# Batch 0's attention in two half batches of plain float32 products, and weights laid out tile by tile

## What is computed

```python
# attention, 8 heads of 64; a query sees itself and the 127 tokens before it
scores = q @ k.T / 8 - slope[h] * |i - j|         # masked outside the window
attn = softmax(scores);  x = concat_heads(attn @ v)            # (4, 576, 512)
# MLP with layer norm and residual
xn = (x - mean) / sqrt(var + 1e-6) * g_ln
x = x + relu(xn @ w_ch1) @ w_ch2                  # 512 -> 2048 -> 512
# gated convolution
h = relu(x @ w_in)                                # 512 -> 1024
out = (h * sigmoid(conv3(h))) @ w_out             # three taps along the tokens
```

## Time and profile before

| | us |
|---|---|
| median of 3 runs (lowest, highest) | 835.75 (835.41, 836.39) |
| span of the profiled execution, first to last instruction | 834.8 |
| the same execution's own time | not recorded apart from its span |
| prologue, to the first product of the MLP | 89.0 |
| stage `first` | 151.7 |
| stages `steady` | 139.1 and 139.8 |
| stage `last` | 104.0 |
| convolution part | 211.2 |
| TensorE busy | 786.3 |
| VectorE busy | 547.0 |
| ScalarE busy | 385.0 |
| GpSimd busy | 171.7 |
| store of x of one batch (`x_spill`), issue to landing | 5.3 |

### The profile page before, as it was taken

The page is one execution under the profiler, slowest core; times in us unless marked ns, Lnnn a source line. Parts: engine busy times, 40 slices in busy tenths (PEclk is TensorE's granted clock), DMA queues, the critical chain, the costliest instruction groups (busy, mean ns, idle before and its releaser), DMA issues.

```text
span 834.8 us, 17035 instructions
## 1 busy us (share of the span) xinstructions
PE 786.3 (94%) x5792; PEld 765.4 (92%) x5792; DVE 547.0 (66%) x1510; ACT 385.0 (46%) x1063; POOL 171.7 (21%) x155
## 2 busy tenths in 40 slices
PE   4776788999999999999999999999999999999998
PEld 3665778999999999998999999999998999999998
DVE  4997677777367777645677754522229887788862
ACT  5775456565224655512556632122235444444442
POOL 4553675211011211101112200021120110111100
PEclk9676799999999999999999999999999999999999
DMA  5441554221122123013121201411312122221101
GB/s 154 106 130 48 156 162 127 60 78 43 58 65 66 38 71 101 8 58 102 29 71 51 86 8 61 134 58 54 89 49 76 31 79 78 78 78 47 59 22 44
DMA packets 64425, 60.81 MB, mean 73 GB/s; under 512 B 23904, under 2 KB 52576, under 8 KB 63840
## 3 DMA queue, kind: packets, MB, share of 16 engines
q1 hardware_dynamic: 64352, 59.87, 24.3%
HBM read 45.69 MB, written 14.16 MB: 72 GB/s over the span
## 4 chain that ended last, share of the span: by engine, by line
PE 69%; DVE 11%; issue 11%; POOL 3%; ACT 2%; DMA 2%; SPq 1%; POOLq 0%; DVEq 0%; ACTq 0%
PE bank L1009 20%; PE bank L1011 19%; PE bank L1010 19%; PE bank L950 4%; PE bank L964 3%; PE bank L980 3%; DVE prob L741 2%; DVE q_st L829 1%; DMA w_stage<-w 1%; DMA q_raw<-qT 1%; DVE ch_stage L741 1%; POOL rstd L482 1%; DVE rows L734 1%; ACT prob L562 1%; DVE rows L736 1%
## 5 line engine op out<-in xcount | busy, mean ns | idle before, releaser
L1009 PE MATMUL bank<-h_hi,wb_hi 128*128 128x288 f32 x512 | 156.9, 306 | 3.1 <-DVE h_lo L798 2.3
L1009 PE MATMUL bank<-xn_hi,wa_hi 128*128 128x288 f32 x512 | 157.0, 307 | 2.7 <-issue 1.4
L1010 PE MATMUL bank<-xn_lo,wa_hi 128*128 128x288 f32 x512 | 152.0, 297 | 0.0
L1011 PE MATMUL bank<-xn_hi,wa_lo 128*128 128x288 f32 x512 | 152.0, 297 | 0.0
L1011 PE MATMUL bank<-h_hi,wb_lo 128*128 128x288 f32 x512 | 151.6, 296 | 0.0
L1010 PE MATMUL bank<-h_lo,wb_hi 128*128 128x288 f32 x512 | 151.5, 296 | 0.0
L798 DVE SCALAR_TENSOR_TENSOR h_lo<-bank,h_hi 128x288 fp32r<-128x288 f32 x128 | 58.1, 454 | 109.8 <-ACT h_hi L594 108.5
L594 ACT ACTIVATE h_hi<-bank 128x288 fp32r<-128x288 f32 x128 | 52.3, 409 | 164.1 <-PE bank L1011 163.1
L1009 PEld LDWEIGHTS bank<-h_hi,wb_hi 128*128 128x128 f32 x512 | 97.1, 190 | 5.2 <-issue 3.9
L1009 PEld LDWEIGHTS bank<-xn_hi,wa_hi 128*128 128x128 f32 x512 | 97.6, 191 | 4.0 <-issue 3.2
L1010 PEld LDWEIGHTS bank<-xn_lo,wa_hi 128*128 128x128 f32 x512 | 97.7, 191 | 0.0
(11 more groups left out here) (95 smaller groups left out, 1752.0 us busy)
## 6 DMA issues: line engine op xcount, KB each, us to landing
k_raw<-kT SPq DMA_DIRECT2D x64, 144.0 KB, 2.8
q_raw<-qT SPq DMA_DIRECT2D x64, 144.0 KB, 2.9
w_stage<-w SPq DMA_DIRECT2D x32, 256.0 KB, 3.0
x_in<-x_spill SPq DMA_DIRECT2D x8, 580.0 KB, 4.3
ch_in<-ch_spill SPq DMA_DIRECT2D x8, 580.0 KB, 5.2
x_spill<-xT SPq DMA_DIRECT2D x4, 1152.0 KB, 5.3
ch_spill<-ch_stage SPq DMA_DIRECT2D x32, 144.0 KB, 1.9
out<-out_stage SPq DMA_DIRECT2D x32, 144.0 KB, 1.8
```

The source lines that it names most:

```text
L1009: nc.tensor.matmul(dst, w_h, a_h, start=start, stop=False)
L1010: nc.tensor.matmul(dst, w_h, a_l, start=False, stop=False)
L1011: last = nc.tensor.matmul(dst, w_l, a_h, start=False, stop=stop)
```

## The change

Only batch 0's attention, the weight layout and who splits weights are changed.

- Batch 0's attention is cut into half c = 0 (320 queries) and half c = 1 (256 queries), each for 8 heads: sixteen half-heads. Score tiles: three with 128, 256 and 192 keys (the last of 64 queries) for c = 0, two with 256 keys for c = 1 (`HTILES`).
- Their products are plain float32: q and k are loaded once, by one transfer (the host lays them side by side as `qkT`), GpSimd multiplies q by 2^(h+1) (`scale_q`), there are no high and low parts; the probabilities are copied out once by ScalarE (`half_pt_copy`), and VectorE copies the 64 x 320 (or 256) outputs into `xT` (`half_x`).
- The prologue holds the half-heads of c = 0, one per unit of its own time, twelve weight tiles, the norm of c = 0 and the scores of the first two half-heads of c = 1 (`EARLY_HALVES`). Sum and reciprocal are made once per half-head.
- Stage `first` begins after that. It now also holds the other half-heads of c = 1, one per 1.7 slots from slot -2.6, then the norm of c = 1 at slot 16, and the attention of batch 1 from slot 13.2, one head per 4.95 slots. Twenty weight tiles follow at one per slot. x of batch 0 is stored at slot 19.
- GpSimd makes the low parts of all 32 weight tiles of the MLP; VectorE keeps half of those of the convolution part.
- `w1` and `w_in` come laid out by the host tile by tile, so that a row of a tile is one run of 2 KB.

```diff
+HT, HT0, HK0 = (320, 256), (0, 320), (0, 192)
+HTILES = ([(128, 0, 0, 128, 128, 0), (128, 128, 0, 256, 0, 128), (64, 256, 128, 192, 0, 384)],
+          [(128, 128, 0, 256, 0, 0), (128, 256, 128, 256, 0, 256)])
+HNT = (3, 2)
+HPROB, HPAD = 640, 576
...
+HPARTS = ([(0, 128, 0, 256, 0), (1, 128, 256, 192, 128), (2, 64, 448, 64, 256)],
+          [(1, 128, 128, 256, 0), (0, 128, 0, 128, 0), (2, 128, 384, 128, 128)])
+HALF_PROLOGUE = {("HS", 0): -0.3, ("HS", 1): -0.28, ("HP", 0): 1.8, ("HO", 0): 2.25}
+HALF_FIRST = {("HS", 0): 0.0, ("HP", 0): 2.3, ("HO", 0): 4.45}
+EARLY_HALVES = 2
+HALF0, HALF_SLOTS = -2.6, 1.7
+NORM_TIMES_PROLOGUE = {("IN", 0): 0.0, ("IN", 1): 0.02, ("IN", 2): 0.04, ("OUT", 0): 0.5, ("OUT", 1): 0.8, ("OUT", 2): 1.1}
+FIRST_NORM_0 = 16.0
+FIRST_HEAD_0, HEAD_SLOTS_0, LAST_NORM_0 = 13.2, 4.95, 59.2
+SMALL = 41
+X_SPILL_AT, LOAD_AT = 19.0, 5.0
+W_PROLOGUE = 12
+FIRST_W, W_SLOTS, W_PACE = 0.9, 0.8, 1.0
+LEAD_GAIN_PROLOGUE = 0.5
...
+        out = half_items(0, 0, 1.0, HALF_PROLOGUE, range(H)) + norm_items(H + 1.75, 0, NORM_TIMES_PROLOGUE)
+        out += half_items(1, H, 1.0, {("HS", 0): -0.3}, range(EARLY_HALVES))
         out += [(W_SLOTS * n + FIRST_W, ("W", n)) for n in range(W_PROLOGUE)]
         return sorted(out, key=lambda x: x[0])
-    out = mlp_groups() + norm_items(FIRST_NORM, 1)
+    out = mlp_groups()
     if kind == "first":
         out += [(0.25 + W_PACE * (n - W_PROLOGUE), ("W", n)) for n in range(W_PROLOGUE, NW1)]
-    if kind in ("first", "steady"):
-        out += head_items(FIRST_HEAD, HEAD_SLOTS) + norm_items(LAST_NORM, 0)
+        halves = half_items(1, HALF0, HALF_SLOTS, HALF_FIRST, range(H))
+        out += [(t, x) for t, x in halves if x[0] != "HS" or x[2] >= EARLY_HALVES]
+        out += norm_items(FIRST_NORM_0, 1) + head_items(FIRST_HEAD_0, HEAD_SLOTS_0) + norm_items(LAST_NORM_0, 0)
+        out += [(X_SPILL_AT, ("X",)), (LOAD_AT, ("LOAD",))]
+    elif kind == "steady":
+        out += norm_items(FIRST_NORM, 1) + head_items(FIRST_HEAD, HEAD_SLOTS) + norm_items(LAST_NORM, 0)
...
+    w1_tiles = w1
...
+        def by_pool(n):
+            return n < NW1 or n % 2 == 1
         def wait_w_split(eng, n):
-            if by_pool(n):
-                eng.wait_ge(w_split_pool, n + 1 if n < W_PROLOGUE else (n + W_PROLOGUE) // 2 + 1)
+            if n < NW1:
...
+            def load_half_qk(c, h):
+                e = half_no(c, h)
+                if e >= 2:
+                    c2, h2 = divmod(e - 2, H)
+                    sp.wait_ge(bank_filled, use_of(0, ("HS", c2, h2, len(HGROUPS[c2]) - 1)) + 1)
+                    sp.nop(nofuse=True)
+                n = S - HK0[1] if c else HT[0]
+                sp.dma_start(half_qk[e % 2][:, :, 0:n], qkT[0, h, :, :, HK0[c]:HK0[c] + n]).then_inc(half_qk_loaded[e % 2], 16)
...
+            def scale_q(c, h):
+                e = half_no(c, h)
+                q = half_qk[e % 2][:, 0, HT0[c] - HK0[c]:HT0[c] - HK0[c] + HT[c]]
+                pool.wait_ge(half_qk_loaded[e % 2], 16 * (e // 2 + 1))
+                nc.gpsimd.tensor_scalar(q, q, 2.0 ** (h + 1), None, ALU.mult).then_inc(half_q_scaled, 1)
...
+            def half_exps(c, h, x):
+                for t, _ in HGROUPS[c][x]:
+                    rows, _, _, keys, _, col = HTILES[c][t]
+                    r = half_rows(c, h) + t
+                    act.wait_ge(half_min, tile_of_half(c, h, t) + 1)
+                    scores = half_prob_of(c, h)[0:rows, col:col + keys]
+                    nc.scalar.activation(scores, scores, ACT.Exp, bias=row_min[0:rows, r:r + 1], scale=-1.0,
+                                         accum_out=row_sum[0:rows, r:r + 1]).then_inc(half_exp, 1)
+            def half_pt_copy(c, h):
+                e = half_no(c, h)
+                act.wait_ge(bank_filled, use_of(0, ("HP", c, h, 0)) + 1)
+                if e >= 2:
+                    c2, h2 = divmod(e - 2, H)
+                    act.wait_ge(bank_filled, use_of(0, ("HO", c2, h2, 0)) + 1)
+                nc.scalar.activation(half_pt[e % 2][:], bank[bank_of(0, ("HP", c, h, 0))][:], ACT.Copy).then_inc(half_pt_ready, 1)
...
+            def half_minima(c, h, x):
+                e = half_no(c, h)
+                src = bank[bank_of(0, ("HS", c, h, x))]
+                dve.wait_ge(bank_filled, use_of(0, ("HS", c, h, x)) + 1)
+                if e == 0 and x == 0:
+                    dve.wait_ge(zeros_ready, 1)
+                    dve.wait_ge(dist_ready, 3)
+                if e >= 3 and x == 0:
+                    c3, h3 = divmod(e - 3, H)
+                    dve.wait_ge(bank_filled, use_of(0, ("HP", c3, h3, 0)) + 1)
+                dve.nop(nofuse=True)
+                for t, at in HGROUPS[c][x]:
+                    rows, _, _, keys, b0, col = HTILES[c][t]
+                    r = half_rows(c, h) + t
+                    ins = nc.vector.tensor_tensor_reduce(
+                        out=half_prob_of(c, h)[0:rows, col:col + keys], in0=src[0:rows, at:at + keys],
+                        in1=dist[0:rows, b0:b0 + keys], scale=-SCALE * 2.0 ** -(h + 1), scalar=BIG, op0=ALU.add, op1=ALU.min,
+                        accum_out=row_min[0:rows, r:r + 1])
+                    ins.then_inc(half_min, 1)
+            def half_normalise(c, h):
+                e, n, r = half_no(c, h), HNT[c], half_rows(c, h)
+                dve.wait_ge(half_exp, tile_of_half(c, h, n - 1) + 1)
+                nc.vector.tensor_scalar_add(row_inv[:, r:r + n], row_sum[:, r:r + n], SUM_EPS).then_inc(half_sum, 1)
+                dve.wait_ge(half_sum, 2 * e + 1)
+                nc.vector.reciprocal(row_inv[:, r:r + n], row_inv[:, r:r + n]).then_inc(half_sum, 1)
+                dve.wait_ge(half_sum, 2 * e + 2)
+                for t in range(n):
+                    rows, _, _, keys, _, col = HTILES[c][t]
+                    probs = half_prob_of(c, h)[0:rows, col:col + keys]
+                    nc.vector.tensor_scalar(probs, probs, row_inv[0:rows, r + t:r + t + 1], None, ALU.mult).then_inc(half_prob, 1)
+            def half_x(c, h):
+                half = D * (h % 2)
+                dve.wait_ge(bank_filled, use_of(0, ("HO", c, h, 0)) + 1)
+                nc.vector.tensor_copy(xT[half:half + D, h // 2, HT0[c]:HT0[c] + HT[c]],
+                                      bank[bank_of(0, ("HO", c, h, 0))][0:D, 0:HT[c]]).then_inc(x_ready, 1)
...
+            def half_scores(c, h, x):
+                e = half_no(c, h)
+                take_bank(0, ("HS", c, h, x))
+                dst = bank[bank_of(0, ("HS", c, h, x))]
+                pe.wait_ge(half_q_scaled, e + 1)
+                for t, at in HGROUPS[c][x]:
+                    rows, q0, k0, keys, _, _ = HTILES[c][t]
+                    last = nc.tensor.matmul(dst[0:rows, at:at + keys], half_qk[e % 2][:, 0, q0:q0 + rows],
+                                            half_qk[e % 2][:, 1, k0:k0 + keys], start=True, stop=True)
+                last.then_inc(bank_filled, 1)
...
+            def half_prob_t(c, h):
+                take_bank(0, ("HP", c, h, 0))
+                dst = bank[bank_of(0, ("HP", c, h, 0))]
+                if c == 0 and h == 0:
+                    pe.wait_ge(identity_ready, 2)
+                    pe.wait_ge(zeros_ready, 4)
+                pe.wait_ge(half_prob, tile_of_half(c, h, HNT[c] - 1) + 1)
+                for t, k0, col in HBLOCKS[c]:
+                    rows, _, _, _, _, pcol = HTILES[c][t]
+                    last = nc.tensor.transpose(dst[:, col:col + rows], half_prob_of(c, h)[0:rows, pcol + k0:pcol + k0 + P],
+                                               ident[0:rows, 0:rows])
+                last.then_inc(bank_filled, 1)
...
+            def half_outputs(c, h):
+                e = half_no(c, h)
+                take_bank(0, ("HO", c, h, 0))
+                dst = bank[bank_of(0, ("HO", c, h, 0))]
+                pe.wait_ge(half_v_loaded[e % 4], 32 * (e // 4 + 1) if c == 0 else 32 * 2 + 16 * (e // 4 - 1))
+                pe.wait_ge(half_pt_ready, e + 1)
+                for i, (j, n, src, cols, col) in enumerate(HPARTS[c]):
+                    last = nc.tensor.matmul(dst[0:D, col:col + cols], half_v[e % 4][0:n, j, :], half_pt[e % 2][0:n, src:src + cols],
+                                            start=i == 0, stop=i == 2, skip_group_check=True)
+                last.then_inc(bank_filled, 1)
...
+        "qkT": np.ascontiguousarray(np.stack([inputs["q"].transpose(0, 1, 3, 2), inputs["k"].transpose(0, 1, 3, 2)], axis=3)),
         "v": np.ascontiguousarray(inputs["v"]),
         "g_ln": np.ascontiguousarray(inputs["moe_g_ln"].reshape(DC, P).T),
-        "w1": np.ascontiguousarray(inputs["moe_w_ch1"]),
+        "w1": np.ascontiguousarray(inputs["moe_w_ch1"].reshape(DC, P, F1, P).transpose(2, 1, 0, 3)).reshape(F1, P, DM),
         "w2": np.ascontiguousarray(inputs["moe_w_ch2"]),
-        "w_in": np.ascontiguousarray(inputs["moe2_w_in"]),
```

(1 more changed line is left out.)

428 lines of the change are left out of this document (268 added, 160 removed).

## The result

The changed kernel takes 871.96 us (871.61 to 872.51) beside 835.62 us for the kernel before in the same runs: a ratio of 1.0427, with an interval of 1.0405 to 1.045. The prediction was 809 and faster; it is wrong by 63 us and in sign. The profiled execution has a span of 870.4 us, 35.6 more than before.

The account below looks back on a forecast made before the run. VectorE was taken to bound the head, with TensorE not far behind; dense TensorE work bounds the rest. MLP 0 starting 36.5 us earlier and ending 26.6 earlier gave 835.75 - 26.6 = 809 us, range 797 to 825.

Parts of the forecast that it names:

- Start of the head: Head: q and k land at about 4.1, scaling ends at 4.8, two score tiles at 6.3 us.
- Pace, 4.1 us: Head: each half-head takes 4.1 us, between 3.5 and 5.6, with VectorE at 3.9.
- 0.8 + 2.4/c: Head: TensorE's time per half-head at clock c: 5.6 us always cold, 4.4 at 0.66, 3.2 warm.
- Cold head: Rival, head: clock at the low level throughout, 5.6 us per half-head, 820 us in all; chance 0.08.
- Shared port: Rival, head: GpSimd's work slows VectorE's normalisations, 6.0 us per half-head, 822 us in all; chance 0.05.
- End of the head and norm: End of head: last half-head's chain 8.0 us, x at 43.0, norm 9.5, MLP 0 begins at 52.5.
- MLP 0, 161.6: MLP 0: 139.1 plus half-heads 19.2, less early scores 1.7, plus 5 losses; ends at 214.1, 26.6 us earlier.
- releases come in time: MLP 0: half-heads' two PSUM banks free in time; 4.8 us period, VectorE's work 3.6, ScalarE's 3.4.
- 5 in all: MLP 0: losses, including some 2 us of low clock, taken as 5 us, between 0 and 12.7.
- All after it is unchanged.: Behind MLP 0: every later stage takes as long as before.
- Layout: MLP 0: 2 KB weight rows worth between nothing and GpSimd's 7.3 us wait; only the smaller loss counted.
- the rival of the two banks: Rival, MLP 0: half-heads stall on two banks; slower above 3.3 us each, 841 at 4, 864 at 7.5; chance 0.05.

Follow-up runs that it names:

- e5: Changed kernel with VectorE's normalisation in the head placed ahead of the copy of the previous half-head's outputs: 869.4 us.
- e10: e6 with half-head scores on all 128 rows, q and k loaded into both halves of the partitions: 855.85 us, ratio 1.0251.
- e14: e12 with 128-row scores: 831.1 us beside 835.47 for the kernel before, ratio 0.9938.
- e6: e5 with the head's transposes of one half-head placed before the scores of a later one on TensorE: 862.15 us, ratio 1.0306.
- e8: Changed kernel with low parts of weight tiles from the thirteenth on made by GpSimd and VectorE in turn: 873.01 us.
- e7: Changed kernel with the norms and batch 1's first head moved apart in MLP 0's plan: 857.79 us, ratio 1.0262.
- e11: Changed kernel with the edits of e6 and e7 together, and the third half-head's q and k loaded earlier: 845.41 us.
- e12: e11 with half-head transposes and outputs in MLP 0 0.2 slots later and their normalisation earlier: 838.73 us, ratio 1.0029.
- e4: Changed kernel with the norm of batch 1's first half begun 2.2 slots earlier (LAST_NORM_0 57.0): 868.86 us.
- e3: Kernel before with only w_ch1 and w_in laid out tile by tile: 835.22 us against 836.76, ratio 0.9982.
- e13: Changed kernel with only the half-head scores put on all 128 rows: 866.93 us.
- e1: Changed kernel with blocks of plain float32 products, bf16 products and float32 transposes put ahead of TensorE's work: 946.5 us, one run.

## Why the prediction was wrong

The prediction's sum was 835.75 - 36.5 + 9.9 = 809. In its own steps:

- **Start of the head.** First minima forecast at 6.3, measured 6.7. But the first transposes were due at 10.4 (6.3 and 4.1 of the chain) and came at 16.6. They stand behind the third half-head's scores in TensorE's order, and the load for those stood behind weight and v loads in the sync queue. 6.2 us lost, of which the chain itself is 1.0 (normalised at 11.4). I counted the transfers and did not follow them in order.
- **Pace, 4.1 us.** Measured 6.9: seven times 2.8 is 19.6 us, the largest error. The step that failed is the clock in 0.8 + 2.4/c: I had c near 0.73 because TensorE would be busier, and it was 0.5. By that formula this is 5.6 in place of 4.1, 1.5 of the 2.8. Passes are longer than columns times four cycles: 2.40 for scores where I had 1.92, outputs 2.06 where I had 1.71; e5's mean of 6.4 against 5.6 makes this 0.8. The ring in VectorE's order, with operations that GpSimd holds up: 0.5 (e5, 6.4 against 6.9). e10 and e14 show 4.0 to 4.4 where the clock is up and the order is mended, and 5.1 to 6.0 where GpSimd's operations hold up the normalisation even then. VectorE works 3.2 per half-head from 20.7 to 69.0 us, under my 3.9, and was not the bound. "Cold head", which had 0.08, gave the right clock and 820 us. It left out the longer passes; that e6 runs at 5.5 to 6.0 is chance, since with the 0.8 filled its sum would be 4.8. "Shared port" (0.05) had a true mechanism as well, but the head's waits for normalisation sum to 3.1 us where it had 13.
- **End of the head and norm.** The last half-head's chain was 0.9 longer than forecast, the norm 8.9 where I had 9.5. Together MLP 0 began 26.1 us later than I said.
- **MLP 0, 161.6.** Measured 188.8, 27.2 over. A half-head's operations cost 2.7 us, not 2.4 (scores 1.06, transposes 0.6, outputs 1.01): 2.4 us. The split of the weights costs nothing (e8). What failed is "releases come in time", and with it the loss of "5 in all": idle time is 17.8 us above batch 1's own stage, and the low clock, for which I had 2, some 12 by the estimate above. I tested the two banks for half-heads alone; the plan also puts a norm and batch 1's heads in them. Moving these apart returns 10.3 us (e7), the order of half-head normalisation 6.1 (e11 to e12). Of the 11.4 that e12 is then still over (173.0), the half-heads' price is 2.4 and 3.1 go with 128-row scores (e14). No run takes the other 6 away. The trace places idle time: TensorE is idle 9.5 us of e12's stage, 7.9 more than in batch 1's, 3.2 of it at the norm's transposes into tokens and 2.7 at the half-heads'.
- **"All after it is unchanged."** 8.0 us lost behind MLP 0: the last norm tiles of batch 1 (`LAST_NORM` was 55.5, `LAST_NORM_0` is 59.2) were moved behind the last product. e4 and e7 show 6.6 to 6.7 of it. I read `LAST_NORM_0` as a constant of the plan and did not ask what stands beside it at the end.
- **Layout.** Worth -1.5 us alone (e3), with an interval from -0.3 to -2.7; I counted nothing but a smaller loss.

Two sums of the prediction don't hold by its own numbers. In the rival of the two banks a stall of 4 us, less the 0.6 already counted, gives 836 and not 841. GpSimd's 3.25 of 4.1 us is 79% of the head, not 73%. Neither moves the forecast.

The rival on the other side, the two banks in MLP 0, had 0.05 and came nearest with 841 to 864. It has the right place and only part of the mechanism: the half-heads' waits there are 7.9 us, 1.0 each, and more lies at the norm and in the clock. I set the point from which it decides at 3.3 us per half-head, 26.6/8. That supposed the whole gain of the head. The head came 26.1 us late, which leaves 0.5 of the 26.6 and a point near zero. The stage's 27.2 over and the 8.0 behind it are then all loss: 809 + 26.1 + 27.2 + 8.0 = 870, beside 872 measured.

What stays open: why a pass of 576 columns takes 2.40 us at the low clock and not 1.92 (at the full clock it takes 1.23 and not 0.96, e14 from 19.21, so it is no fixed time); what exactly lets the clock rise in the half-heads. The runs show that in three orders of work it rose in the head with 128 rows and never with 64: e13 against the changed kernel, e10 against e6, e14 against e12. The edit also doubles two small transfers and GpSimd's rows, which no run parts from it. I haven't tried a version with full outputs.

## What to carry to other kernels

Taking work off the busiest engine pays only down to the next limit. Here that was TensorE's own chain at the low clock, and close beside it a ring of waits. Before pricing the new pace, add up the next engine's work at the low clock, then write down each engine's order for one period and follow the ring across engines, the copy in front of the normalisation included. Don't count on the clock rising because an engine gets busier. When work moves into a full stage, list everything that shares its buffers there (here a norm and two heads in two banks), not only the moved work. Price each risk against a reduced gain too: the head's loss alone (26.1 us) or MLP 0's alone (27.2) would have left the time near that of before, 835 or 836, and all together made it 36 us slower.

## What the runs showed of the hardware

- A plain float32 product of 256 columns takes 0.431 us at the full clock, one bf16 product 0.113, and it takes 0.435 with 64 rows or with 64 stationary columns: half a product costs the same.
- 150 float32 transposes of 128x128 back to back pass every 0.110 us at the full clock, which stays up for the 16.5 us they take (e1).
- From 12 to 57 us of e12 TensorE worked nearly without idle time (waits of 0.40 and 0.78) and stayed at the low clock, on half-heads whose scores use 64 rows; with 128 rows in the scores (e14), otherwise the same order, it was at the full level from about 18 to 29 and from about 39 to 50 us.
- The clock row of the page can show the full level while durations are those of the low level: transposes of 1.3 us in the head of the changed kernel (granted clock 1.00 from 0 to 78.6 us) beside 0.78 in e10, and 1.27 there where the row shows 0.5.
